# Up-projections of two channel mixers as seven block products for eight, woven between the down-projections

## Chip, cores, metric

One core of one Trainium2 chip. The metric is the device time of one execution in microseconds (us). Before the change it is 791.82 us, median of 3 executions (791.28 to 792.13).

## What is computed

`x` is the output of a clustered attention, 2 batches of 768 tokens with 512 features. Two mixer layers follow, each a token mixing and a channel mixing. All of it is float32.

```python
def _moe_ref(x, U, V, w_ch1, w_ch2):            # layer 1: w_ch1 512 x 2048, w_ch2 2048 x 512
    xt = x.transpose(0, 2, 1)
    h = xt @ U @ V
    u = x + h.transpose(0, 2, 1)
    ch = np.maximum(u @ w_ch1, 0.0) @ w_ch2
    return (u + ch).astype(np.float32)

def _moe2_ref(x, w_tok1, w_tok2, w_ch1, w_ch2): # layer 2: w_ch1 512 x 1536, w_ch2 1536 x 512
    xt = x.transpose(0, 2, 1)
    h = np.maximum(xt @ w_tok1, 0.0) @ w_tok2   # 768 -> 256 -> 768
    u = x + h.transpose(0, 2, 1)
    h2 = np.maximum(u @ w_ch1, 0.0) @ w_ch2
    return (u + h2).astype(np.float32)
```

## The kernel before

Everything runs in a format of TensorE with a reduced mantissa (`F32R`), so each operand is split into a high part (ScalarE, a copy that rounds) and a low part (VectorE, the value minus its high part), and each product is three matmuls: high by high, high by low, low by high. Engines are programmed one by one, each with its own instruction list, and meet only in semaphores (`wait_ge`, `then_inc`), so the order within an engine is the order in which its list is written.

`attention` fills the first 266 us or so. `mixers` (L774) does the rest. `x` stays in SBUF as 12 tiles of 128 tokens by 512 features, the first six those of batch 0. PSUM has eight banks: `hid` (2), `spare` (2), `acc` (4).

**Tokens.** `token_first(L)` (L944, matmuls L957) contracts over tokens; `token_second(L, i)` (L961, L976) brings tile i back to tokens, and VectorE adds it to x (L1117). In layer 1, VectorE first makes the low parts of batch 1's tiles (L1099). GpSimd (POOL) splits V and the two token weights (L906 to L919), and between the layers it splits x (L926, L928).

**Channels.** `channel(L)` (L979) goes over three chunks of 512 tokens. Four tiles are transposed on TensorE (L940) and split out of PSUM by ScalarE (L1043) and VectorE (L1094). Then come the hidden features, one tile f of 128 at a time: `up(f)` (L984, L989) is 4 feature tiles x 3 = 12 matmuls with 512 moving columns into one of two `hid` banks; ScalarE takes relu and the high part out of PSUM (L1067), VectorE the low part (L1126); `down(f)` (L993, L998) is 4 token tiles x 3 = 12 matmuls of 512 columns that accumulate in `acc` over all f. The order is up(f+1), down(f), up(f+2), and so on. The weights of tile f are loaded by SyncE (L882, L884) and split by ScalarE (L1039, L1069) and VectorE (L1089, L1130). At the end of a chunk VectorE adds `acc` to x (L1150). There are 84 pairs of a chunk and a tile f (3 x 16 and 3 x 12), so 1008 up matmuls and 1008 down matmuls. The loops over f are hardware loops.

Of the kernel before, what the change touches and what calls it, by code (L numbers as in the profile page):

```python
# [4 lines left out]
F32 = mybir.dt.float32  # L5
F32R = mybir.dt.float32r
I32 = mybir.dt.int32
ALU = mybir.AluOpType
# [765 lines left out]
def mixers(nc, x, hi, q_lo, ident, V_raw, uv_in, w_ch1, w_ch2, w_tok1, w_tok2, v_ch1, v_ch2, out):  # L774


    R2 = w_tok1.shape[1]
    NR = R2 // P
    NTT = B * NT
    TPC = CHUNK // P  # L780
    layers = [(w_ch1, w_ch2), (v_ch1, v_ch2)]
    with ExitStack() as ctx:
        def sb(name, shape, dt=F32):
            return ctx.enter_context(nc.sbuf_tensor(name, shape, dt))
# [4 lines left out]


        bank = [ctx.enter_context(nc.psum_tensor(f"bank{i}", [P, BANK], F32)) for i in range(8)]
        hid, spare, acc = bank[0:2], bank[2:4], bank[4:8]


        x_hi, x_lo = token_tiles(hi[0]), token_tiles(hi[1])
        uT_hi = [sb(f"uT_hi{i}", [P, KD, CHUNK], F32R) for i in range(2)]
        uT_lo = [sb(f"uT_lo{i}", [P, KD, CHUNK], F32R) for i in range(2)]
        w1_raw = [sb(f"w1_raw{i}", [P, KD, P]) for i in range(2)]
        w2_raw = [sb(f"w2_raw{i}", [P, DM]) for i in range(2)]
        w1_hi = [sb(f"w1_hi{i}", [P, KD, P], F32R) for i in range(2)]  # L800
        w1_lo = [sb(f"w1_lo{i}", [P, KD, P], F32R) for i in range(2)]
        w2_hi = [sb(f"w2_hi{i}", [P, DM], F32R) for i in range(2)]
        w2_lo = [sb(f"w2_lo{i}", [P, DM], F32R) for i in range(2)]
        h_hi = [sb(f"h_hi{i}", [P, CHUNK], F32R) for i in range(2)]
        h_lo = [sb(f"h_lo{i}", [P, CHUNK], F32R) for i in range(2)]


        U_st = q_lo[:, 0, :].rearrange("p (t c) -> p t c", t=NT)
        V_hi = q_lo[:, 1, :]
        V_lo = q_lo[:, 2, :]  # L810
        t1 = sb("t1", [4 * RANK, B, DM], F32R)

        wt1_raw = sb("wt1_raw", [P, NT, R2])
        wt1_hi, wt1_lo = (q_lo[:, at:at + 2, :].rearrange("p g s -> p (g s)").rearrange("p (t r) -> p t r", t=NT)
                          for at in (4, 6))
        wt2_raw = sb("wt2_raw", [P, NR, S])
        wt2_hi = sb("wt2_hi", [P, NR, S], F32R)
        wt2_lo = sb("wt2_lo", [P, NR, S], F32R)
        t2_hi = sb("t2_hi", [P, B * NR, DM], F32R)
        t2_lo = sb("t2_lo", [P, B * NR, DM], F32R)  # L820
# [3 lines left out]
        wt_made = sem("wt_made")  # L824
        w1_in = [sem(f"w1_in{i}") for i in range(2)]
        w2_in = [sem(f"w2_in{i}") for i in range(2)]
        w1_hi_made = sem("w1_hi_made")
        w1_made = sem("w1_made")
        w2_hi_made = sem("w2_hi_made")
        w2_made = sem("w2_made")  # L830
        h_hi_made = sem("h_hi_made")
        h_made = sem("h_made")
        uT_hi_made = sem("uT_hi_made")
        uT_made = sem("uT_made")
        x_hi_made = sem("x_hi_made")
        x_made = sem("x_made")
        hid_mm = sem("hid_mm")
        acc_mm = sem("acc_mm")
        y_made = sem("y_made")
# [5 lines left out]
        u_tr = sem("u_tr")  # L845
        out_stored = sem("out_stored")


        nf = [layers[L][0].shape[1] // P for L in range(2)]
        chunks = [(L, c) for L in range(2) for c in range(NCHUNK)]  # L850
        base = [sum(nf[l] for l, _ in chunks[:i]) for i in range(len(chunks))]
        TOKS = (B, B * NR)
# [4 lines left out]
        def bank_of(L, n):  # L857

            return spare[n] if L == 0 or n < NR else hid[n - NR]

        def transposed_tile(a, i):
            cc, k = i // TPC, i % TPC
            return a[cc % 2][:, :, k * P:(k + 1) * P]

        def on_chip_order(a, t0=0):
            return a.rearrange("r (p t) -> r t p", t=NT)
# [3 lines left out]

        block = ctx.enter_context(nc.Block())

        @block.sync
        def _(sp):
            for L, (wa, wb) in enumerate(layers):
                wa3 = wa.rearrange("(k p) f -> p k f", p=P)
                for c in range(NCHUNK):
                    n0 = base[L * NCHUNK + c]

                    def load(f, par):  # L880
                        wait(sp, w1_made, n0 + f - 1)
                        sp.dma_start(w1_raw[par][:, :, :], wa3[:, :, bass.ds(f * P, P)]).then_inc(w1_in[par], 16)  # L882
                        wait(sp, w2_made, n0 + f - 1)
                        sp.dma_start(w2_raw[par][:, :], wb[bass.ds(f * P, P), :]).then_inc(w2_in[par], 16)  # L884

                    load(0, 0)
                    load(1, 1)
                    if L == 0 and c == 0:
                        sp.dma_start(wt1_raw[:, :, :], w_tok1.rearrange("(p t) r -> p t r", t=NT)).then_inc(wt_in[0], 16)
                        sp.dma_start(wt2_raw[:, :, :], w_tok2.rearrange("(n p) s -> p n s", p=P)).then_inc(wt_in[1], 16)  # L890
                    with sp.Fori(0, nf[L] // 2 - 1) as i:
                        load(i * 2 + 2, 0)
                        load(i * 2 + 3, 1)
                    if L == 1 and c == NCHUNK - 1:

                        out_v = out.rearrange("b (p t) d -> b p t d", t=NT)
                        for i in range(NTT):
                            sp.wait_ge(y_made, NTT + i + 1)
                            sp.dma_start(out_v[i // NT, :, i % NT, :], tile_of(x, i)).then_inc(out_stored, 16)
# [301 lines left out]
```

## Time and profile before

| | |
|---|---|
| median of 3 executions | 791.82 us (791.28 to 792.13) |
| the profiled execution | 792.6 us |
| span of its profile | 790.7 us |
| TensorE (PE) busy | 768.8 us |
| VectorE (DVE), ScalarE (ACT), GpSimd (POOL) busy | 450.1, 361.7, 136.0 us |

The profile is of one execution. [...] PEld is the load of weights into the array. "Idle before" is the time for which an engine stood still ahead of a group. PEclk is the granted TensorE clock, 1.00 for 2.4 GHz and 0.50 for 1.2 GHz. Tensors that share an address are printed under one name of theirs (`kT_hi` in L1099 is `x_lo`, `qT_lo` in L908 is `V_lo`).

### The profile page before, as it was taken

The numbers are of one execution on the slowest core, as the hardware profiler recorded it, in microseconds if no ns is written. First come the engines' busy times: TensorE is split into PE (matmuls) and PEld (weight loads), VectorE is DVE, ScalarE is ACT, GpSimd is POOL, SyncE is SP. The second block draws the span as 40 slices with busy tenths as digits, with TensorE's granted clock in tenths as the row PEclk, the third lists the DMA queues.
The fourth block names the chain that finished last, engine by engine and source line by source line (L and its number), as shares of the span: only waits on it lengthen the run. The fifth ranks groups of instructions, "written<-read, shape, count | busy, mean of one in ns | idle before, by whom it ended". The sixth has DMA issues, their size and how long they took to land.

```text
span 790.7 us, 12902 instructions
## 1 busy us (share of the span) xinstructions
PE 768.8 (97%) x3997; PEld 659.8 (83%) x3997; DVE 450.1 (57%) x761; ACT 361.7 (46%) x742; POOL 136.0 (17%) x162
## 2 busy tenths in 40 slices
PE   7989999999999889999999999999999999999998
PEld 6878999999999668888888888888888888888886
DVE  4778999999999684333533353334254335334333
ACT  5567888888888533323333233332123233323321
POOL 1351332233228660000300040000300000000000
PEclk9999999999999999999999999999999999999999
DMA  7935354444441223333323323333003333333334
GB/s 246 225 105 134 94 122 103 119 105 119 105 117 33 70 96 101 93 105 83 104 80 106 99 84 110 88 98 106 0 1 107 93 93 94 93 106 84 103 105 173
DMA packets 82840, 81.08 MB, mean 103 GB/s; under 512 B 7296, under 2 KB 69056, under 8 KB 82816
## 3 DMA queue, kind: packets, MB, share of 16 engines
q1 hardware_dynamic: 82816, 80.77, 37.0%
q8 instruction: 14, 0.23, 0.1%
q14 instruction: 10, 0.08, 0.0%
HBM read 56.95 MB, written 4.72 MB: 78 GB/s over the span
## 4 chain that ended last, share of the span: by engine, by line
PE 63%; DVE 2%; ACT 0%; issue 0%
PE bank L998 29%; PE bank L989 29%; PE bank L976 2%; PE bank L957 2%; PE bank L940 1%; DVE kT_hi L1099 1%; DVE x L1117 0%; DVE x L1150 0%; DVE w_lo L1130 0%; DVE uT_lo L1094 0%; DVE w_lo L1089 0%; DVE t L1108 0%; DVE h_lo L1126 0%; ACT qT_hi L1048 0%; ACT h_hi L1067 0%
## 5 line engine op out<-in xcount | busy, mean ns | idle before, releaser
L1126 DVE SCALAR_TENSOR_TENSOR h_lo<-bank,h_hi 128x512 fp32r<-128x512 f32 x84 | 58.1, 692 | 261.8 <-ACT h_hi L1067 261.8
L1067 ACT ACTIVATE h_hi<-bank 128x512 fp32r<-128x512 f32 x84 | 50.2, 598 | 301.4 <-PE bank L989 301.4
L989 PE MATMUL bank<-uT_hi,w_hi 128*128 128x512 f32 x336 | 131.2, 391 | 0.0
L998 PE MATMUL bank<-w_hi,h_hi 128*128 128x512 f32 x336 | 131.1, 390 | 0.0
L989 PE MATMUL bank<-uT_hi,w_lo 128*128 128x512 f32 x336 | 130.8, 389 | 0.0
L989 PE MATMUL bank<-uT_lo,w_hi 128*128 128x512 f32 x336 | 130.8, 389 | 0.0
L998 PE MATMUL bank<-w_hi,h_lo 128*128 128x512 f32 x336 | 130.7, 389 | 0.0
L998 PE MATMUL bank<-w_lo,h_hi 128*128 128x512 f32 x336 | 130.7, 389 | 0.0
L595 DVE TENSOR_TENSOR pT_lo<-back,pT_hi 128x384 fp32r<-128x384 f32 x192 | 98.1, 552 | 6.9 <-ACT pT_hi L496 3.5
L496 ACT ACTIVATE pT_hi<-back 128x384 fp32r<-128x384 f32 x192 | 84.4, 497 | 36.2 <-PE back L740 34.6
L563 DVE TENSOR_REDUCE negmax<-front 128x1 f32<-128x768 f32 x96 | 91.3, 952 | 9.2 <-PE front L639 9.2
L447 ACT ACTIVATE prob<-front,negmax 128x768 f32<-128x768 f32 x96 | 87.9, 916 | 1.2 <-DVE negmax L563 1.2
L740 PE MATMUL back<-ident,prob 128*128 128x128 f32 x576 | 79.3, 274 | 0.4 <-DVE pT_lo L595 0.4
L989 PEld LDWEIGHTS bank<-uT_hi,w_hi 128*128 128x128 f32 x336 | 63.1, 188 | 13.5 <-DVE uT_lo L1094 0.4
L998 PEld LDWEIGHTS bank<-w_hi,h_hi 128*128 128x128 f32 x336 | 63.1, 188 | 13.2 <-issue 0.2
L998 PEld LDWEIGHTS bank<-w_hi,h_lo 128*128 128x128 f32 x336 | 63.1, 188 | 13.1
L989 PEld LDWEIGHTS bank<-uT_hi,w_lo 128*128 128x128 f32 x336 | 63.0, 188 | 13.1
L989 PEld LDWEIGHTS bank<-uT_lo,w_hi 128*128 128x128 f32 x336 | 63.1, 188 | 12.9
L998 PEld LDWEIGHTS bank<-w_lo,h_hi 128*128 128x128 f32 x336 | 63.1, 188 | 12.9
L740 PEld LDWEIGHTS back<-ident,prob 128*128 128x128 f32 x576 | 68.4, 141 | 2.7 <-DVE pT_lo L595 0.6
L758 PE MATMUL back<-pT_hi,v_split 128*128 128x384 f32 x192 | 67.9, 354 | 0.8 <-DVE pT_lo L595 0.6
L760 PE MATMUL back<-pT_lo,v_split 128*128 128x384 f32 x192 | 64.8, 337 | 0.0
(125 smaller groups left out, 1054.1 us busy)
## 6 DMA issues: line engine op xcount, KB each, us to landing
w_raw<-in_moe_w_ch_dram SPq DMA_DIRECT2D x168, 256.0 KB, 2.9
Q<-qT_hi SPq DMA_DIRECT2D x64, 96.0 KB, 2.2
K<-kT_hi SPq DMA_DIRECT2D x64, 96.0 KB, 2.1
q_raw<-in_q_dram SPq DMA_DIRECT2D x8, 384.0 KB, 6.0
k_raw<-in_k_dram SPq DMA_DIRECT2D x8, 384.0 KB, 7.0
Q<-qT_lo SPq DMA_DIRECT2D x32, 96.0 KB, 2.1
K<-kT_lo SPq DMA_DIRECT2D x32, 96.0 KB, 2.1
v_raw<-in_v_dram SPq DMA_DIRECT2D x16, 192.0 KB, 2.7
```

What stands on the lines that cost most here:

```text
L447: nc.scalar.activation(prob[t % 2][:, :], s_slot[t % 2], ACT.Exp, bias=negmax[:, t % TPP:t % TPP + 1], accum_out=sums[:, t % TPP:t % TPP + ...
L496: nc.scalar.activation(pT_hi[G % 2][:, HT * half:HT * half + HT, P * (t % GT):P * (t % GT) + P], t_bank[n % 3][:, 0:HT * P].rearrange("p ( ...
L563: nc.vector.tensor_reduce(negmax[:, t % TPP:t % TPP + 1], s_slot[t % 2], AX.X, ALU.max, negate=True).then_inc(max_done, 1)
L595: nc.vector.tensor_tensor(pT_lo[G % 2][own], t_bank[n % 3][:, 0:HT * P].rearrange("p (n c) -> p n c", c=P), pT_hi[G % 2][own].bitcast(F32) ...
L740: last = nc.tensor.transpose(t_bank[i % 3][:, t * P:(t + 1) * P], prob[n % 2][:, c:c + P], ident[:, :])
L758: nc.tensor.matmul(av_bank, v_sp[j][:, token_of(t), :], pT_hi[n % 2][:, t, :], start=(t == 0), stop=False)
L760: last = nc.tensor.matmul(av_bank, v_sp[j][:, token_of(t), :], pT_lo[n % 2][:, t, :], start=False, stop=(t == NT - 1))
L957: last = nc.tensor.matmul(bank_of(L, n)[:, :], w, y[:, i, :], start=(t == 0 and m == 0), stop=(t == NT - 1 and m == len(pairs) - 1))
L989: last = nc.tensor.matmul(hid[par][:, :], w[par][:, kd, :], y[cc % 2][:, kd, :], start=(kd == 0 and m == 0), stop=(kd == KD - 1 and m == 2))
L998: last = nc.tensor.matmul(acc[k][:, :], y[par][:, k * P:(k + 1) * P], w[par][:, :], start=(start and m == 0), stop=(stop and m == 2))
L1067: nc.scalar.activation(h_hi[par][:, :], hid[par][:, :], ACT.Relu).then_inc(h_hi_made, 1)
L1126: nc.vector.scalar_tensor_tensor(out=h_lo[par][:, :], in0=hid[par][:, :], scalar=0.0, in1=h_hi[par][:, :].bitcast(F32), op0=ALU.max, op1=A ...
```

## The change

The channel mixers work on four chunks of 768 tokens, one for each layer and batch (`cc` 0 to 3), and on pairs of hidden tiles (8, 8, 6 and 6 pairs, 28 in all; n is the pair's number in all of them, p that in its chunk). For one pair, the up-projection is a 2 x 2 by 2 x 2 block product: weights in halves of the features and two hidden tiles, activations in halves of the features and halves of the tokens (384 columns). It is formed with seven block products in place of eight (Winograd's form of Strassen's scheme), each of 2 x 3 = 6 matmuls of 384 columns.

- The weight sums (four, 128 x 256) are made by GpSimd (`pair_sums`), the activation sums (four, 128 x 768) by VectorE at the start of each chunk (`moving_sum`), between adding the last chunk's result to x (`settle`) and making low parts (`moving_low`, seven of 128 x 768 for a chunk).
- The products' results are put together by VectorE with seven adds of 384 columns (`combine`), each of a PSUM bank and something in SBUF; one product is first copied by ScalarE (`snapshot`). The hidden values now lie in SBUF (`h`), and are split from there with 768 columns at a time.
- Only two banks (`hid`) are left for products, so product q waits until q - 2 has been read; six banks are `acc`. After product q (1 to 6) of pair p come two of the twelve down units (3 matmuls each) of pair p - 1. A chunk's first pair has no pair before it; the last pair's down units run among the next chunk's transposes.
- Layer 2's token mixing of a batch is woven into the first two pairs of chunks 1 and 2 (`MIXED`), with x split by ScalarE and GpSimd (`stage_high`, `stage_low`).
- Every list is written out in full, without hardware loops. Many tensors of the mixers lie over attention's or each other's.

The diff, cut to its core (the removed side is the code above); first the constants, the wait for a bank, and GpSimd's list:

```diff
+    PRODS, COMBS, RING = 7, 7, 3
+    A_SLOT = (0, 1, 5, 2, 4, 6, 3)
+    READ_BY = (0, 1, 2, 3, 5, 6, 7)
+    BC_SUM = {2: 2, 3: 3, 4: 1, 6: 4}
+    UNITS = [(e, k) for e in range(2) for k in range(NT)]
+    MIXED = (1, 2)
+        acc, hid = bank[0:NT], bank[NT:]
...
+        def product_read(eng, n, q):
+            if q == 0:
+                eng.wait_ge(snap_done, n + 1)
+            else:
+                eng.wait_ge(comb_done, COMBS * n + READ_BY[q])
...
+            def pair_sums(n):
+                raw = a_raw[n % 2]
+                pool.wait_ge(w1_in[n % 2], (n // 2 + 1) * 32)
+                nc.gpsimd.tensor_tensor(raw[:, 4, :, :], raw[:, 2, :, :], raw[:, 3, :, :], ALU.add).then_inc(sums_made, 1)
...
+            def stage_low(m):
+                pool.wait_ge(st_hi_made, m + 1)
+                nc.gpsimd.tensor_tensor(x_lo[:, m % RING, :], tile_of(x, m), x_hi[:, m % RING, :].bitcast(F32),
+                                        ALU.subtract).then_inc(st_made, 1)
...
+            pair_sums(0)
...
+            pool.wait_ge(tok_mm, B)
+            for r in range(NR):
+                nc.gpsimd.tensor_copy(tiled(wt2_hi[:, r, :]), on_chip_order(wt2_raw[:, r, :])).then_inc(wt2_made, 1)
...
+            pair_sums(1)
+            for n in range(pbase[NCH]):
+                for cc in MIXED:
+                    if n == pbase[cc]:
+                        for t in range(NT):
+                            stage_low((cc - 1) * NT + t)
+                if n + 2 < pbase[NCH]:
+                    pair_sums(n + 2)
```

TensorE's list, after `token_second_low` and the first transposes:

```diff
+            for cc in range(NCH):
+                for p in range(npair[cc]):
+                    for q in range(PRODS):
+                        product(cc, p, q)
+                        if p > 0 and q > 0:
+                            down(cc, p - 1, 2 * q - 2)
+                            down(cc, p - 1, 2 * q - 1)
+                        if (cc, p, q) == (0, 0, 1):
+                            for t in range(NT // 2, NT):
+                                token_second_low(1, t)
+                        if cc in MIXED and p == 0 and q > 1:
+                            token_first(cc, q - 2)
+                            if q == PRODS - 1:
+                                token_first(cc, NT - 1)
+                        if cc in MIXED and p == 1 and q == 0:
+                            for t in range(NT):
+                                token_second(cc, t)
+                more = cc + 1 < NCH
+                for unit in range(len(UNITS)):
+                    if more and unit == 0:
+                        transpose_u(cc + 1, 0)
+                    if more and unit < NT - 1:
+                        transpose_u(cc + 1, unit + 1)
+                    down(cc, npair[cc] - 1, unit)
```

VectorE's list, after the low parts of batch 1's tiles, of `t1`, and six `add_mix`:

```diff
+            for part in range(2):
+                a_low(0, part)
+            for cc in range(NCH):
+                for p in range(npair[cc]):
+                    if p == 0:
+                        moving_low(cc, 0)
+                        moving_low(cc, 1)
+                        dve.wait_ge(uT_made, NT * (cc + 1))
+                        down_read(dve, n - 2, 1)
+                        moving_sum(cc, tmp2, block_of(0, 1), block_of(0, 0))
+                        dve.wait_ge(bc_sum, 4 * cc + 1)
+                        moving_sum(cc, tmp1, block_of(1, 1), tmp2)
+                        moving_sum(cc, block_of(0, 1), block_of(1, 1), block_of(0, 1))
+                        settle(cc, 0)
+                        moving_low(cc, 2)
+                        settle(cc, 1)
+                        moving_low(cc, 3)
+                    elif p == 1 and mixed:
+                        for t in range(NT):
+                            add_mix(cc + 1, t)
+                    combine(n, 1, c11, snap)
+                    combine(n, 2, c12, snap)
+                    if p == 0:
+                        dve.wait_ge(bc_made, PRODS * cc + 3)
+                        moving_sum(cc, tmp1, block_of(1, 0), tmp1)
+                        settle(cc, 2)
+                        moving_low(cc, 4)
+                    else:
+                        for e in range(2):
+                            w2_low(n, e)
+                        if more:
+                            a_low(n + 1, 0)
+                    combine(n, 3, c21, c12, 2)
+                    if p == 0:
+                        settle(cc, 3)
+                        moving_low(cc, 5)
+                    elif more:
+                        a_low(n + 1, 1)
+                    combine(n, 4, c22, c21, 3)
+                    combine(n, 4, c12, c12, 2)
+                    if p == 0:
+                        settle(cc, 4)
+                        moving_low(cc, 6)
+                        settle(cc, 5)
+                        for part in range(2):
+                            a_low(n + 1, part)
+                    combine(n, 5, c12, c12, 5)
+                    if p == 0:
+                        for e in range(2):
+                            w2_low(n, e)
+                    h_low(n, 0)
+                    combine(n, 6, c21, c21, 3)
+                    h_low(n, 1)
+                    if p == 0 and mixed:
+                        for r in range(NR):
+                            t2_low(cc, r)
```

Product q waits for `bc_made` (its moving low part) in a chunk's first pair, for `a_made` (both `a_low` of its pair) at q = 0, and for `product_read` of q - 2. ScalarE's list in a chunk's first pair is: six copies out of the transposes' banks with two `moving_high` after the third, then `moving_high` 2 to 6 with the snapshot after number 3, `stage_high` of six tiles among them in a mixed chunk (tile t after `settle` t), `a_high` of the next pair, the two `w2_high`, the two `h_high`, and in a mixed chunk `t2_high` twice. `token_second` waits for both `t2_low`.

## Rows read from the trace of the kernel before

**Rows 1.** Page, part 1: busy us and share by engine.

```profile
PE 768.8 (97%) x3997; PEld 659.8 (83%) x3997; DVE 450.1 (57%) x761; ACT 361.7 (46%) x742; POOL 136.0 (17%) x162
```

**Rows 2.** Chain that ended last, in order of time: start us, us, what.

```profile
298.64 2.72 PE bank L989 x12
...
380.24 0.87 PE bank L940 x8
...
553.48 16.32 PE bank L957 x72
```

**Rows 3.** Timeline of PE and PEld, attention's last group of 384 columns: start, us.

```profile
263.62 0.34 PE L760 MATMUL back<-pT_lo,v_split 128*128 128x384 f32 x1
263.62 0.19 PEld L758 LDWEIGHTS back<-pT_hi,v_split 128*128 128x128 f32 x1
...
265.38 0.33 PE L760 MATMUL back<-pT_lo,v_split 128*128 128x384 f32 x1
```

**Rows 4.** The same chain as in rows 2, from the mixers' start.

```profile
269.76 6.57 DVE kT_hi L1099 x6
...
279.09 3.68 DVE x L1117 x6
...
291.61 2.29 DVE w_lo L1130
...
295.87 2.77 PE bank L998 x12
```

**Rows 5.** Timelines of DVE, POOL, ACT, mixers' start and 470 to 473 us: start, us.

```profile
269.09 1.65 POOL L906 CAST qT_lo<-V_raw 128x768 fp32r<-128x768 f32 x1 [0.34 <-POOLq L95]
269.76 1.53 DVE L1099 TENSOR_TENSOR kT_hi<-x,qT_hi 128x512 fp32r<-128x512 f32 x1 [3.37 <-ACT qT_hi L1048]
270.82 2.55 POOL L908 TENSOR_TENSOR qT_lo<-V_raw,qT_lo 128x768 fp32r<-128x768 f32 x1
271.21 2.71 DVE L1099 TENSOR_TENSOR kT_hi<-x,qT_hi 128x512 fp32r<-128x512 f32 x1
275.31 0.63 ACT L1039 ACTIVATE w_hi<-w_raw 128x512 fp32r<-128x512 f32 x1 [0.87 <-DMA w_raw<-in_moe_w_ch_dram]
...
470.37 1.14 DVE L1130 TENSOR_TENSOR w_lo<-w_raw,w_hi 128x512 fp32r<-128x512 f32 x1
470.91 1.07 POOL L926 CAST qT_hi<-x 128x512 fp32r<-128x512 f32 x1
471.44 1.09 DVE L1089 TENSOR_TENSOR w_lo<-w_raw,w_hi 128x512 fp32r<-128x512 f32 x1
472.06 1.62 POOL L928 TENSOR_TENSOR kT_hi<-x,qT_hi 128x512 fp32r<-128x512 f32 x1
472.48 0.69 DVE L1126 SCALAR_TENSOR_TENSOR h_lo<-bank,h_hi 128x512 fp32r<-128x512 f32 x1
```

**Rows 6.** Groups by line and shape: xcount | busy us, mean ns | idle before.

```profile
L595 DVE TENSOR_TENSOR pT_lo<-back,pT_hi 128x384 fp32r<-128x384 f32 x192 | 98.1, 552 | 6.9 <-ACT pT_hi L496 3.5
L1089 DVE TENSOR_TENSOR w_lo<-w_raw,w_hi 128x512 fp32r<-128x512 f32 x84 | 57.5, 690 | 7.2 <-ACT w_hi L1039 7.2
L569 DVE SCALAR_TENSOR_TENSOR qT_lo<-back,qT_hi 128x768 fp32r<-128x768 f32 x8 | 7.6, 954 | 5.2 <-ACT qT_hi L465 5.2
L447 ACT ACTIVATE prob<-front,negmax 128x768 f32<-128x768 f32 x96 | 87.9, 916 | 1.2 <-DVE negmax L563 1.2
L385 POOL TENSOR_TENSOR avsum<-av 128x192 f32<-128x192 f32 x32 | 19.1, 598 | 130.9 <-ACT av L503 130.9
L913 POOL TENSOR_TENSOR qT_lo<-wt_raw,qT_lo 128x1536 fp32r<-128x1536 f32 x1 | 3.5, 3481 | 0.1
L919 POOL TENSOR_TENSOR wt_lo<-wt_raw,wt_hi 128x768 fp32r<-128x768 f32 x2 | 4.5, 2257 | 0.2
```

**Rows 7.** Windows: us, busy (x) of PE, PEld, DVE, ACT, POOL, PEclk, DMA.

```profile
266.00:269.00 3.00, 0.55 (x3) 0.31 (x3) 0.39 (x2) 0.49 (x1) 1.09 (x2) 1.00 0.00 0
270.30:273.60 3.30, 3.30 (x9) 2.58 (x9) 3.30 (x2) 2.03 (x4) 2.99 (x2) 0.52 0.59 183
```

More of the change, by code:

```diff
@@ new lines, in mixers @@
+        uT = sb("uT", [P, KD, S])
+        sb("wt1_area", [P, KD, S])
+        with ExitStack() as under:
+            sb("bc_area", [P, 2 * PRODS - 2, 2, GW], where=under)
+            wt2_raw = sb("wt2_raw", [P, NR, S], where=under)
+        bc_hi = sb("bc_hi", [P, PRODS, 2, GW], F32R)
+        bc_lo = sb("bc_lo", [P, PRODS, 2, GW], F32R)
+        with ExitStack() as under:
+            tmps = []
+            for n in range(2):
+                tmps.append(sb(f"moving_sum{n}", [P, 2, GW], where=under))
+                sb(f"moving_area{n}", [P, 2 * DM - 2 * GW], where=under)
@@ new lines, in flat_a, with rows @@
+        def flat_a(a):
+            return a[:, :, :, :].rearrange("p s k c -> p (s k c)")
+        def rows(a, first, count):
+            return a[:, first:first + count, :].rearrange("p n c -> p (n c)")
+        tmp2, tmp1 = (t[:, :, :] for t in tmps)
+        snap = V_raw[:, 0:GW]
+        V_hi, V_lo = (flat_a(a_hi[1])[:, i * S:(i + 1) * S] for i in range(2))
+        t1 = flat_a(a_lo[1])[:, 0:B * DM].rearrange("p (b c) -> p b c", b=B)
+        t2_hi, t2_lo = (a[:, RING:RING + NR, :] for a in (x_hi, x_lo))
@@ L874, in _ @@
         def _(sp):
[L875 to L899, printed above, removed]
@@ new lines, in token_second @@
+            def token_second(cc, t):
+                cols = slice(t * P, (t + 1) * P)
+                m = (cc + 1) * NT + t
+                ring = NT - NR
+                if t == 0:
+                    pe.wait_ge(wt2_made, 2 * NR)
+                    pe.wait_ge(tok_made, B + NR * cc)
+                    pe.wait_ge(y_made, cc * NT)
+                wait(pe, u_made, m - ring + 1 if t >= ring else 0)
+                for r in range(NR):
+                    for i, (w, y) in enumerate(((wt2_hi, t2_hi), (wt2_hi, t2_lo), (wt2_lo, t2_hi))):
+                        last = nc.tensor.matmul(acc[NR + t % ring][:, :], w[:, r, cols], y[:, r, :],
+                                                start=(r == 0 and i == 0), stop=(r == NR - 1 and i == 2))
+                last.then_inc(mix_mm, 1)
@@ L1153, in program @@
+            for k in range(NT):
+                add_down(NCH - 1, k)
 def program(nc, q, k, v, centroids, U, V, w_ch1, w_ch2, w_tok1, w_tok2, v_ch1, v_ch2, out):
```

581 lines of the change are left out of this document (335 added, 246 removed).

## Prediction

> **What bounds the kernel now.** I read the page's busy times first: TensorE is busy for 97% of the span, and the next engine for 57% [rows 1]. Then the chain of waits, in order of time: from 295.87 us to the end it is TensorE alone, 12 matmuls in 2.72 us again and again (226.7 ns for each 512 columns), eight transposes in 0.87 us (0.11 each), the written-out 72 matmuls of L957 at the same full pace (16.32 us) [rows 2]. So only fewer or shorter matmuls help, as long as nobody makes TensorE wait. The one part that TensorE does not set is the mixers' start: 26.8 us from 269.1 to the first down matmul at 295.87 [rows 4], holding 48 token matmuls (10.9 us), 24 up matmuls (5.4) and 32 transposes (3.5), 19.8 us of work. VectorE holds most of that chain [rows 4]. The change puts four such seams where there is one.
>
> **The saving.** Columns of 384 appear in attention: ten starts from 263.62 to 265.38 us, 176 ns each, though each has a weight load of 190 ns of its own [rows 3]. Up-projection before: 1008 x 226.7 ns = 228.5 us. After: 28 pairs x 7 products x 6 = 1176 matmuls x 176 ns = 207.0 us. **Saved: 21.5 us.** Down, token and transpose matmuls keep their numbers (1008, 192, 96). [...]
>
> **Prices.** VectorE takes 3.68 us for six adds of 512 in a row, 0.61 each [rows 4]; one alone lasts 0.55, 0.69 and 0.95 us at 384, 512 and 768 columns [rows 6]. In a row I take 0.64 for 512 with its wait, 0.9 for 768, 2.0 for the two `a_low` (1792 columns together), 0.55 for a `combine`. ScalarE takes 0.92 for 768 [rows 6]. GpSimd goes from 0.60 us at 192 columns to 3.48 at 1536 [rows 6], so by that line 0.75 for one weight sum of 256, 3.1 for a pair's four with their waits, 1.3 for a `stage_low`.
>
> **The lock.** A two-input VectorE instruction from SBUF waits while GpSimd works. L1099's first lasts 1.53 us beside the V_hi cast and its second 2.71, ending half a microsecond after V_lo; at 470 us they take turns: 1.14 and 1.09 us for VectorE instructions whose group has a mean of 0.69, with GpSimd's 1.07 and 1.62 between and after them. L1126, which reads PSUM, takes 0.69 beside a running GpSimd subtraction [rows 5, 6]. Before, most of VectorE's work in a seam reads PSUM. After, `moving_low`, `moving_sum`, `a_low`, `w2_low` and `h_low` all read SBUF twice. [...] The rows show turns.
>
> **Opening, chunk 0.** Six VectorE subtractions end at 276.33 [rows 4]; the four sums of `pair_sums(0)` now fall among the last of them, once the weights land at about 275 (the third load of before released ScalarE at 275.31 [rows 5]), and take two turns: 277.8. Then `t1` (no longer behind two `w1_low`) and six `add_mix`: 283.5. From there VectorE's list up to the first down matmul, if it never waited: two `a_low` 2.0; `moving_low` 0 to 6, 6.3; four `moving_sum` 3.6; six `settle` 3.9; six `combine` of pair 0 (q = 1 to 5, two of them for q = 4), 3.3; two `a_low` 2.0; two `w2_low` 1.3; `h_low` 0.9; `combine` 6, 0.55: 23.9 us, to 307.4, and product 1 of pair 1 (1.05) ends at 308.5. Meanwhile GpSimd has the rest of `wt1_lo` (3), the two casts and two subtractions of `wt2` (1.65 and 2.26 each, 7.8 in all [rows 5, 6]), and the sums of pairs 1 and 2 (6.2): 17 us, each instruction between two of VectorE's. Some 3.5 us of it lie beside `settle` and `combine`, which read PSUM. That leaves 13.5: **first down matmul at 322**. TensorE's work by then is 10.9 + 24 transposes 2.6 + 9 products 9.5 = 23.0 us. Beyond its work it takes 322 - 269.1 - 23.0 = 29.9 us, before 7.0. **Cost 22.9 us**; bounds 9.5 (GpSimd never in the way) and 27 (all of its time counts).
>
> **Chunks 1 and 2.** Count from the last pair's transposes, which alternate with its down units: TensorE is through with both at 11.2 us (24 x 0.11 + 36 x 0.2267 = 10.8, and 0.4 for two waits for copies). `uT` is complete at about 6.7, because two `moving_high` (0.9 each) stand between ScalarE's copies. From 6.7 VectorE needs: four sums 3.6, five `moving_low` 4.5, six `settle` 3.9, six `combine` 3.3, two `a_low` 2.0: 17.3, with 0.5 of waits for products 24.5. Six `stage_low` (1.3 each, 7.8) lie there too; half find PSUM work beside them: 28.4. TensorE fills the time with 7 products (7.4) and 36 `token_first` matmuls (8.2), to 26.8, so it waits some 1.6 us. After one more product, at 29.5, it stands before `token_second`, which waits for `t2_low`: VectorE still has two `w2_low`, `h_low`, `combine` 6 (2.8), `pair_sums` of the next pair take turns with them (3.1), then `h_high` 0.9, two `t2_high` 1.2 and the last `t2_low` 0.7: 36.4 to 37.1. What is late next is that one wait, and behind it nothing on TensorE can go. **Cost 8.3 us each**, 16.6; bounds 3.3 (no lock) and 11 each.
>
> **Chunk 3.** No token matmuls, no GpSimd work in the list: 24.5, then `w2_low`, `h_low`, `combine` 6 to 27.3, product 1 to 28.4. TensorE's nine products (9.5) fit in the 17.2 us after 11.2. **Cost 7.7**; bounds 6 and 10.
>
> **Inside a chunk.** A pair takes 42 x 0.176 + 36 x 0.2267 = 15.6 us. VectorE needs 7 x 0.55 + 1.3 + 2.0 + 1.8 = 9.0, with all of GpSimd's 3.1 before it 12.1; between a product and the one that wants its bank lie two units and a product (2.4 us), where `combine` needs 0.55 behind at most three other instructions. I cost it at nothing; its cover is those 3.5 us. SyncE issues `load_pair` of n + 2 after `a_low` of n and `load_w2` of n, in pair n - 1, so a pair ahead of GpSimd's use; at 15.6 us a pair nothing there either. Written-out code: the 72 matmuls of L957 are written out and run at full pace [rows 2]. The tail (last adds paced by units of 0.68 us) stays.
>
> **Clock.** TensorE was busy for 0.55 of 3 us, and then ran 3.3 us at a granted 0.52 (1.2 GHz) although busy throughout [rows 7]. Nine matmuls ran where full pace has 14.6, a loss of some 1.6 us. The seams' waits can do the same: once each in chunks 1 and 2, one and a half times in the opening, where a slow product is mostly hidden by VectorE. **Cost 4 us**, bounds 0 and 7.
>
> **Sum.** -21.5 + 22.9 + 16.6 + 7.7 + 4 = +29.7 on the profiled execution's 792.6, that is 822.3. It was 0.8 us above the median, so 821.5, some 3.7% slower.
>
> **Rivals.**
> - *GpSimd does not hold VectorE up* (it is served second, or its work falls into gaps). Then -21.5 + 9.5 + 6.6 + 6 + 0 to 2 = +1 to +3 us, 793 to 795, up to 800 with half of the lock. For it: L1126 and the other PSUM reads go untouched, and a GpSimd instruction between two waits of VectorE costs nothing; against it: the turns in rows 5. Chance 0.17, a third of it within 0.2%.
> - *Faster: the seams cost less than the saving.* It is decided at one point, the sum of the four seams' waits against 21.5 us. If VectorE ran its SBUF list at a third less than my prices, opening +5, chunks 1 and 2 +1 each, chunk 3 +4 give -10.5: 781. Against: 0.95 us for 768 columns in a row of 8 [rows 6]. For: the two mixed chunks have 8.2 us of token matmuls to fill in. Chance 0.14.
> - *Inside a chunk, too, a product waits for its bank*, because `combine` stands behind `w2_low` and `a_low` and these behind GpSimd. Half of the slack missed in 24 woven pairs, 1 us each: 846. Chance 0.08.
> - *The 384-column matmul gains nothing here*, its weight load of 190 ns being the pace: 1176 x 190 = 223, saving 5: 838. Rows 3 speak against it. Chance 0.03.
>
> My forecast keeps 0.58. Its own range is 805 to 836. Down to 787 it takes in the first rival, up to 838 a part of the others; about 2 in 10 is left out, most of it the faster rival. Faster or slower by 0.2% (1.6 us, about what a measurement of this kernel can tell) counts as a change: faster 0.15, same 0.06, slower 0.79.
>
> **What would show it.** In the changed kernel: products' matmuls start 176 ns apart; inside a chunk TensorE runs without gaps, 15.6 us a pair; the first down matmul stands near 322 us; in VectorE's groups the two-input SBUF instructions of the seams last longer than 0.95 us on average, those that read PSUM do not; `token_second` has the longest single waits, for `t2_low`; the clock dips after them. The forecast is wrong if the first down matmul stands before 310, if the waits before `token_second` are under 3 us, or if gaps appear inside chunks.

## The result, and the profile after

The changed kernel takes **819.39 us** (median of 4 executions, 816.92 to 822.90) against 791.98 (791.28 to 793.95) beside it: a ratio of **1.0345, 95% interval 1.0302 to 1.0389**. The profiled execution took 820.13 us, span 818.2, mean granted clock 0.970. The forecast was 821.5 and "slower".

The first parts of the page, to be laid beside [rows 1]:

```profile
PE 767.1 (94%) x4165; PEld 684.9 (84%) x4165; DVE 579.1 (71%) x893; ACT 386.0 (47%) x698; POOL 234.2 (29%) x262
```

TensorE's work hardly changed in busy time (768.8 before), since its recorded spans overlap (343 to 347 ns on average for a matmul of 384 columns, 173.6 from start to start) and some matmuls now run at half clock (granted 0.50); VectorE has 129 us more, GpSimd 98. What matters is where TensorE stands still. Its waits in the whole kernel, with total, number and longest (L1087 are the products, L1053 is `token_second`):

```profile
PE bank L1087 <- DVE bc_lo L1279: 12.8, 7, 3.8
PE bank L1053 <- issue: 10.8, 2, 5.4
PE bank L1087 <- DVE h L1299: 5.4, 4, 1.8
```

Products wait for `moving_low` (L1279) or for `combine` (L1299), the token matmuls twice for 5.4 us; "issue" means that the view names no releaser there.

**Inside a chunk** the chain of waits is TensorE alone: six matmuls of a product, six of two down units, in turn, and twelve where two products meet.

```profile
333.84 2.08 PE bank L1087 x12
335.92 1.39 PE bank L1101 x6
337.31 1.04 PE bank L1087 x6
...
349.48 2.08 PE bank L1087 x12
```

From 333.84 to 349.48 is one pair: 15.64 us. Before, two hidden tiles of 512 tokens took 4 x 2.72 us, and for 768 tokens that is 4 x 2.72 x 1.5 = 16.32 [rows 2]. The twelve matmuls of 384 columns take 2.083 us, 173.6 ns each.

**The opening.** Mixers start at 268.20 (the first split of a batch 1 tile, at 269.1 before [rows 4]); the first down matmul is at 318.42, 50.2 us later, against 26.8 before and 52.9 forecast. The chain of waits there, beginning and end:

```profile
268.89 8.17 DVE kT_hi L1303 x6
...
279.23 3.68 DVE x L1253 x6
282.91 4.58 DVE a_lo L1245 x2
287.49 5.11 DVE bc_lo L1279 x2
292.60 2.90 DVE moving_sum L1273
...
299.82 2.30 PE bank L1087 x6
...
305.66 2.30 PE bank L1087 x6
...
316.13 2.29 PE bank L1087 x6
318.42 2.56 PE bank L1101 x6
```

The first row is the subtractions that took 6.57 us in [rows 4]. `a_low` (L1245) takes 4.58 for two, two `moving_low` 5.11, one `moving_sum` (L1273) 2.90; the prediction had 2.0, 1.8 and 0.9. Three products take 2.30 us each, at half clock (granted 0.50 at all three), in place of 1.05. The order of time of both engines says why (start, length, instruction; the rows of the other engines are left out):

```profile
280.66 3.49 POOL L991 TENSOR_TENSOR qT_lo<-h,qT_lo 128x1536 fp32r<-128x1536 f32 x1
282.83 4.66 DVE L1245 TENSOR_TENSOR a_lo<-a_raw,a_hi 128x1024 fp32r<-128x1024 f32 x2
...
284.10 2.56 POOL L995 CAST qT_hi<-wt_raw 128x768 fp32r<-128x768 f32 x1
...
286.75 2.78 POOL L997 TENSOR_TENSOR kT_hi<-wt_raw,qT_hi 128x768 fp32r<-128x768 f32 x1
287.41 5.19 DVE L1279 TENSOR_TENSOR bc_lo<-uT,bc_hi 128x768 fp32r<-128x768 f32 x2
...
289.47 2.31 POOL L995 CAST qT_hi<-wt_raw 128x768 fp32r<-128x768 f32 x1
...
291.86 2.81 POOL L997 TENSOR_TENSOR kT_hi<-wt_raw,qT_hi 128x768 fp32r<-128x768 f32 x1
292.52 2.97 DVE L1273 TENSOR_TENSOR moving_sum<-uT 128x768 f32<-128x768 f32 x1
```

From 282.83 us on the ends of the two engines' records alternate, one of GpSimd's and one of VectorE's: GpSimd's at 284.15, 286.66, 289.53, 291.78 and 294.67, VectorE's at 285.24, 287.49, 290.34, 292.60 and 295.49. That is what this document calls turns. The two `moving_low` last 5.19 us (2.93 and 2.34) beside a subtraction of 2.78 and a cast of 2.31; each ends 0.8 us after the GpSimd instruction that was running when it started, and in chunk 3, with GpSimd idle, the same two take 1.83 us. The groups by shape show which instructions stretch:

```profile
L1299 DVE TENSOR_TENSOR h<-bank,h 128x384 f32<-128x384 f32 x140 | 75.0, 552 | 51.3 <-PE bank L1087 51.2
L1279 DVE TENSOR_TENSOR bc_lo<-uT,bc_hi 128x768 fp32r<-128x768 f32 x16 | 19.3, 1226 | 5.4 <-ACT bc_hi L1162 5.4
L1279 DVE TENSOR_TENSOR bc_lo<-moving_sum,bc_hi 128x768 fp32r<-128x768 f32 x12 | 11.3, 945 | 0.0
L1273 DVE TENSOR_TENSOR moving_sum<-uT 128x768 f32<-128x768 f32 x4 | 5.8, 1461 | 2.4 <-ACT uT L1152 2.4
```

Two SBUF inputs: up to 1461 ns on average (of the four first `moving_sum`, the opening's takes 2966 ns, the median is 959), and 945 in the group that does not stretch; in chunk 3, where GpSimd has nothing from 705 to 724 us, each alone takes 0.94 to 0.96 us and two in a row 1.83. One input in PSUM: 552, as before [rows 6].

**The mixed seam** of chunk 1 (chunk 2's is the same), from product (n+1, 0) on, in the chain of waits:

```profile
454.87 1.05 PE bank L1087 x6
455.92 5.39 issue
461.31 10.51 PE bank L1053 x36
```

and TensorE by stretches across it (after the stretch: length, busy time and count of PE, PEld, DVE, ACT and POOL, then the granted clock, DMA share, GB/s):

```profile
457.00:460.40 3.40, 0.00 (x0) 0.00 (x0) 2.49 (x4) 2.23 (x5) 1.25 (x1) 0.77 0.89 235
460.40:463.80 3.40, 2.49 (x6) 2.04 (x7) 0.80 (x2) 2.59 (x3) 2.34 (x4) 0.50 0.04 12
463.80:467.20 3.40, 3.40 (x12) 2.65 (x12) 1.38 (x2) 0.00 (x0) 0.50 (x1) 0.72 0.00 0
```

TensorE stands still for 5.4 us and comes back at a granted 0.50. There its matmuls of 512 columns start 0.427 us apart (461.87 to 464.86), in the opening's slow products those of 384 start 0.320 apart (300.31 to 301.91), both 1.2 columns a ns; at 1.00 the step from 384 columns (173.6 ns) to 512 (226.7) is 53.1 ns, 2.4 columns a ns. Counted as one column a cycle, these are the 1.2 and 2.4 GHz of the sections ahead. The 36 matmuls behind the wait take 10.51 us, in the second seam 10.90, where 36 x 0.2267 = 8.16 at the upper level in an unbroken row.

**Where the 27.5 us went**, from one profiled execution (792.6) to the other (820.13):

| term | forecast | measured |
|---|---|---|
| narrower matmuls | -21.5 | -21.5, and +1.5 (below) |
| mixers start | 0 | -0.9 |
| opening | +22.9 | +20.2 |
| chunks 1 and 2 | +16.6 | +12.4 of waits |
| chunk 3 | +7.7 | +8.2 |
| clock, outside the opening | +4 | +1.8 behind the opening, 2.4 and 2.7 behind the mixed waits |
| not placed | | +0.7 |
| sum | +29.7 | +27.5 |

The opening's 20.2 is 50.2 less 23.0 of work, against 7.0 before. A mixed seam's 6.2 is 461.31 - 427.67 (its first transpose), less 27.4 of work, and chunk 3's 8.2 is 28.56 less 20.3; the forecast had counted 0.4 us of waits for copies as work in each, so on its own terms each of these three seams is 0.4 smaller. Half-clock time lies inside the opening too, in its 20.2. VectorE is busy beside the first two slow products and stands still for 0.45 us at the end of each; nothing runs beside the third (2.29 for 1.05). That makes 2.1 us at most.

### The profile page after: what moved, and what is told of

Its sections match the earlier page's. It is cut to its first block, busy times and chain, and to the rows that moved or that the text cites. A ratio compares the mean times of both kernels' runs of the same rounds, so it can differ in the third digit from the quotient of the medians.

```text
span 818.2 us, 12517 instructions
## 1 busy us (share of the span) xinstructions
PE 767.1 (94%) x4165; PEld 684.9 (84%) x4165; DVE 579.1 (71%) x893; ACT 386.0 (47%) x698; POOL 234.2 (29%) x262
## 4 chain that ended last, share of the span: by engine, by line
PE 56%; DVE 8%; issue 3%; POOL 0%; ACT 0%; ACTq 0%
PE bank L1101 28%; PE bank L1087 23%; PE bank L1053 3%; DVE bc_lo L1279 2%; DVE h L1299 1%; PE bank L1069 1%; DVE a_lo L1245 1%; DVE kT_hi L1303 1%; DVE x L1258 1%; DVE x L1253 1%; DVE moving_sum L1273 1%; PE bank L1038 0%; POOL kT_hi L979 0%; DVE w_lo L1284 0%; DVE kT_hi L1289 0%
## 5 line engine op out<-in xcount | busy, mean ns | idle before, releaser
L1087 PE MATMUL bank<-bc_hi,a_hi 128*128 128x384 f32 x392 | 136.1, 347 | 18.2 <-DVE bc_lo L1279 12.8
L1087 PE MATMUL bank<-bc_lo,a_hi 128*128 128x384 f32 x392 | 135.3, 345 | 0.0
L1087 PE MATMUL bank<-bc_hi,a_lo 128*128 128x384 f32 x392 | 134.4, 343 | 0.0
L1101 PE MATMUL bank<-w_hi,kT_hi 128*128 128x512 f32 x336 | 133.7, 398 | 0.0
L1101 PE MATMUL bank<-w_lo,qT_hi 128*128 128x512 f32 x336 | 133.0, 396 | 0.0
L1101 PE MATMUL bank<-w_hi,qT_hi 128*128 128x512 f32 x336 | 132.6, 395 | 0.0
L1299 DVE TENSOR_TENSOR h<-bank,h 128x384 f32<-128x384 f32 x140 | 75.0, 552 | 51.3 <-PE bank L1087 51.2
L1087 PEld LDWEIGHTS bank<-bc_hi,a_hi 128*128 128x128 f32 x392 | 76.0, 194 | 29.7 <-DVE bc_lo L1279 15.9
L563 DVE TENSOR_REDUCE negmax<-front 128x1 f32<-128x768 f32 x96 | 91.2, 951 | 9.0 <-PE front L639 9.0
L1087 PEld LDWEIGHTS bank<-bc_lo,a_hi 128*128 128x128 f32 x392 | 76.2, 194 | 7.2
L1087 PEld LDWEIGHTS bank<-bc_hi,a_lo 128*128 128x128 f32 x392 | 76.1, 194 | 0.0
L1101 PEld LDWEIGHTS bank<-w_hi,kT_hi 128*128 128x128 f32 x336 | 63.3, 188 | 13.5
L1299 DVE TENSOR_TENSOR h<-bank,V_raw 128x384 f32<-128x384 f32 x56 | 31.2, 557 | 55.8 <-PE bank L1087 55.8
```

Source lines behind the costliest of these rows:

```text
L563: nc.vector.tensor_reduce(negmax[:, t % TPP:t % TPP + 1], s_slot[t % 2], AX.X, ALU.max, negate=True).then_inc(max_done, 1)
L1087: last = nc.tensor.matmul(up_bank(n, q), w[n % 2][:, A_SLOT[q], kt, :], y[:, q, kt, :], start=(kt == 0 and i == 0), stop=(kt == 1 and i == 2))
L1101: last = nc.tensor.matmul(acc[k][:, :], y[:, e, k * P:(k + 1) * P], w[n % 2][:, e, :], start=(start and i == 0), stop=(stop and i == 2))
L1299: nc.vector.tensor_tensor(dst, up_bank(n, q), other, ALU.add).then_inc(comb_done, 1)
```

## The experiments

Two theories stood against each other for each seam. **A**: the time is VectorE's list, lengthened by turns with GpSimd's instructions, and the place of what TensorE waits for in that list. **B**: it is something else, the list's length alone, TensorE's own work, or the clock. The mixers' start moves between executions, from 268.2 to 273.1 us, although all before it is the same code. From the 17th of attention's 96 row maxima (VectorE, L563) to the last is 174.8 to 174.9 us in every trace, and the 17th starts between 81.9 and 86.9 us, so the difference arises before it. So lengths are also given from the mixers' start to the end of the span: 521.6 before, 550.0 after. Ratios are to the kernel before.

### Take GpSimd's split of the second token weight away

```diff
-            for r in range(NR):
-                nc.gpsimd.tensor_copy(tiled(wt2_hi[:, r, :]), ...)
-                ...
-                nc.gpsimd.tensor_tensor(tiled(wt2_lo[:, r, :]), ..., ALU.subtract)...
```

> Left out: GpSimd's two casts and two subtractions of the second token weight in the opening (10.5 us as recorded in the changed kernel, 7.8 us alone), so layer 2's second token product uses leftovers. Theory (GpSimd and VectorE take turns, each GpSimd instruction stands between two of VectorE's): the first down matmul, at 318.4 us in the changed kernel, comes 6 to 8 us earlier, 311.5, and the whole about as much, 812 to 813. Rival (the opening is VectorE's own list, GpSimd costs nothing): the first down matmul stays within 1 us, and the time with it.

812.73 us, ratio 1.0250 (1.0221 to 1.0279). The first down matmul is at 312.81, 42.9 after the mixers' start at 269.94: **7.3 less**, which A had at 6 to 8. From the start, 540.1. Four GpSimd instructions of 10.5 us in all, none of which anyone on TensorE waits for before `token_second`, cost 7 us of the opening. Most of the other 2.6 us of the 9.9 since the start is clock: here the matmuls right behind the opening run at the full one (the first six down matmuls take 1.39 us at a granted 1.00, not 2.56 at 0.50).

### The same time on GpSimd, without SBUF reads

```diff
+            for r in range(NR):
+                for i in range(6):
+                    wait(pool, wt2_made, 6 * r + i)
+                    nc.gpsimd.memset((wt2_hi if i < 3 else wt2_lo)[:, r, :].bitcast(F32), 0.0)...
```

> GpSimd's four instructions for the second token weight are twelve fills of 768 columns instead (some 8 us, as long as the four were alone), which write SBUF and read nothing; layer 2's second token product then uses zeros. Theory (what takes turns is reading SBUF, not GpSimd's being busy): VectorE's two moving_low of the opening take 1.8 us in place of 5.1, and the first down matmul comes 6 to 8 us earlier, as where the four were left out. Rival (GpSimd's being busy, or the semaphores that its list reaches late, hold VectorE): no change against the changed kernel.

813.93 us, ratio 1.0271 (1.0247 to 1.0295); first down 41.4 us after the start, not later than without any split (42.9). The order of time, GpSimd and VectorE:

```profile
283.39 2.33 POOL L997 MEMSET qT_hi<- 128x768 f32 x3
283.62 2.08 DVE L1244 TENSOR_TENSOR a_lo<-a_raw,a_hi 128x1024 fp32r<-128x1024 f32 x2
...
285.62 1.82 DVE L1278 TENSOR_TENSOR bc_lo<-uT,bc_hi 128x768 fp32r<-128x768 f32 x2
...
285.78 2.33 POOL L997 MEMSET kT_hi<- 128x768 f32 x3
```

GpSimd is about as busy (four times 2.33 us), and two `moving_low` take 1.82 us instead of 5.19. So it is not GpSimd's being busy that holds VectorE here but its instructions that read SBUF: a `moving_low`, with its two SBUF inputs, takes 0.91 us beside fills against 2.6 beside casts and subtractions.

### Late settle, alone

In chunks 0 and 3, which have no token mixing, the six `settle` follow the last `combine` of the first pair instead of standing between the `moving_low`, and each of the first down units waits for its own `settle` only.

```diff
-                        settle(cc, 0)   # ... settle(cc, 5), between the moving_low
+                        if mixed:
+                            settle(cc, 0)
...
+                    for k in range(2, NT if late else 2):
+                        settle(cc, k)
```

> Only the late settle of chunks 0 and 3, in the changed kernel. Theory (list length): the six adds of 0.6 us leave the path but the first: in chunk 3 the first down matmul comes 3.3 us earlier (25.3 us behind the first transpose in place of 28.6). In chunk 0 less, since settle also lay beside GpSimd's turns, 0 to 3 us. 813 to 816 in all. Rival (products, not VectorE, set the seam): no change.

815.61 us, ratio 1.0283 (1.0260 to 1.0306). The first down matmul comes 46.1 us after the start (-4.1, expected 0 to -3), and chunk 3's 26.35 after its first transpose (-2.2, expected -3.3). VectorE's list is the limit in chunk 3 too, where GpSimd has nothing, but only from its first `combine` on. That one waits for product 1, in the changed kernel for 1.19 us and here for 2.25:

```profile
715.42 0.56 DVE L1299 TENSOR_TENSOR h<-bank,V_raw 128x384 f32<-128x384 f32 x1 [1.19 <-PE bank L1087]
712.80 0.56 DVE L1302 TENSOR_TENSOR h<-bank,V_raw 128x384 f32<-128x384 f32 x1 [2.25 <-PE bank L1087]
```

(the first row is the changed kernel's, the second this run's). The two `settle` ahead of it filled a wait for TensorE and had cost nothing; of the four behind it, 0.6 us each, 2.2 us come back.

### GpSimd's sums later in the mixed seams

```diff
                 if n + 2 < pbase[NCH]:
+                    for cc in MIXED:
+                        if n == pbase[cc]:
+                            pool.wait_ge(tok_made, B + NR * cc)
                     pair_sums(n + 2)
```

> In chunks 1 and 2 GpSimd makes the weight sums of the pair after next only when t2_low is through. Theory (turns): the wait ahead of token_second, 5.4 us twice, shrinks by the 3.1 us of the four sums to about 2.3 each; 6 us in all, 813. If the shorter wait also keeps the clock up, another 2.7 us for each. Rival (the wait is VectorE's and ScalarE's own chain of w2_low, h_low, combine, h_high, t2_high, t2_low): no change.

816.09 us, ratio 1.0301 (1.0259 to 1.0342). The wait is 4.2 us instead of 5.4: **-1.2, not -3.1**. The turns with the sums were a smaller part of this wait than I had it; the next run shows that the order of the lists is the larger. The matmuls behind the wait took 10.03 and 9.85 us. From the start the run is 4.9 us shorter, of which the two waits are 2.4; much of the rest is clock, here and behind the opening, whose code is the same.

### `t2` first in both lists

ScalarE makes `t2_high` ahead of `h_high`, VectorE `t2_low` ahead of `h_low` and the last `combine`; the sums wait as above.

```diff
-                        if mixed:            # ScalarE: h_high, then t2_high
+                    if mixed and p == 0:     # t2_high, then h_high
+                        for r in range(NR):
+                            t2_high(cc, r)
```

> In chunks 1 and 2 the two t2_high stand before h_high and the two t2_low before h_low, and GpSimd's sums of the pair after next wait for them. Theory (token_second waits for a chain that is late only by its place in the lists): the wait of 5.4 us goes to about 1, and the half clock behind it (2.7 us) goes with it, some 7 us for each, 805 to 807. Rival (the work put off comes back as a wait of the product behind token_second, and the clock falls anyway): 4 us or less for each, 811 or more.

809.26 us, ratio 1.0201 (1.0175 to 1.0228), above the 805 to 807 that A had. From the start, 536.75: **-13.2**, near A's 7 for each seam.

```profile
456.31 1.00 issue
457.31 2.76 PE bank L1056 x11
```

The wait is 1.0 us, and the 36 matmuls behind it take 8.43 us in both seams. Against 5.4 and 10.51 or 10.90, the place in the lists cost, with the sums' 1.2, 4.4 us of waiting and 2.1 to 2.5 of clock in each.

### Fill the wait with matmuls that nobody uses

```diff
                         if cc in MIXED and p == 1 and q == 0:
+                            for i in range(20):
+                                nc.tensor.matmul(acc[NT - 1][:, :], wt1_hi[:, i % NT, 0:P], ...)
```

> Twenty matmuls of 512 columns without use (4.5 us) ahead of each token_second, inside its wait of 5.4 us, into a bank that the next matmul there starts anew. Theory (the half clock behind the wait costs time of its own): the 36 matmuls of token_second take 8.2 us in place of 10.9, 2.7 us less each, 814 in all. Rival (the clock costs nothing that is not waited for anyway): no change within 1 us; if the fill ends after t2_low, up to 1 us slower each.

817.33 us, ratio 1.0299 (1.0268 to 1.0330), where 814 was expected; from the start 545.7, -4.3.

```profile
454.94 4.57 PE bank L1133 x20
459.51 0.81 issue
460.32 8.44 PE bank L1053 x36
```

`token_second` starts no earlier against the seam's own beginning (22.49 us after the down matmuls' end, as without them), but its 36 matmuls take **8.44 us instead of 10.51, and 8.43 instead of 10.90** in the second, at a granted 1.00 in both. The only thing that differs is what TensorE did before: 4.57 us of matmuls in place of standing still. So the clock is a cost of its own, 2.1 and 2.5 us (A had 2.7), and the wait is not TensorE's to shorten. The 0.27 us by which 8.43 exceeds 8.16 is not the clock's; the table's 2.4 and 2.7 hold it.

What the clock takes behind such a wait varies. Over all the runs of this document:

| wait before `token_second` | its 36 matmuls, us |
|---|---|
| 0.8 to 1.0 | 8.42 to 8.44 |
| 2.3 | 10.04, 10.05 |
| 4.2 | 9.85 to 11.27 |
| 5.3 to 5.4 | 9.79 to 11.23 |

A wait of 2.3 us already costs 1.6 us of clock, and one of 5.4 between 1.4 and 2.8.

### The first `a_low` of the next pair at the end of the last

```diff
-                        for part in range(2):
-                            a_low(n + 1, part)
+                        if cc == 0:
+                            ...
+                    if p == npair[cc] - 1 and cc + 1 < NCH:
+                        for part in range(2):
+                            a_low(n + 2, part)
```

> The low parts of a chunk's second pair of weights are made before the seam's activation work, while VectorE waits for the transposes (chunks 1 to 3). Theory (the seam is VectorE's list): chunk 3's first down matmul, 28.6 us behind its first transpose, comes 2.0 us earlier; in chunks 1 and 2, where a_low took 3.7 us in turns with GpSimd, 2 to 3.7; 6 to 9 us in all, 811 to 813. Rival (the seam is set by the products' order or by ScalarE's copies, which now start later): no change, or 1 us slower for each seam.

806.78 us, ratio 1.0162 (1.0132 to 1.0192), below the 811 to 813 that were expected. The four executions lie far apart, from 802.98 us (granted clock 0.985) to 814.60 (0.973), and the profile is of the slowest; from its start, 541.1, -8.9, inside the 6 to 9. Two us of VectorE's list less give 1.8 in chunk 3, and 3.1 of the wait in each mixed seam (2.28 for 5.39), more than they last alone; in the changed kernel they take 3.72 in the first mixed seam, in turns with GpSimd's work. ScalarE's high parts move along with them and now delay the seam's second transposes, so against the first transpose `token_second` comes 2.8 us earlier.

### All sums on VectorE: a miss

`pair_sums` moves from GpSimd to VectorE, 0.34 us a sum.

> All weight sums on VectorE (four of 256 columns, about 1.4 us a pair with waits) in place of GpSimd (3.1 us alone). Theory (turns): the opening loses 6.2 us of GpSimd turns and gains 1.4, first down matmul at 313 to 314; the waits ahead of token_second lose 3.1 us each; inside a chunk nothing changes, VectorE has 10.4 of 15.6 us. In all about 11 us less, 808. Rival (only VectorE's own list counts): 1.4 us more in the opening and in no place less, 820 to 822.

818.87 us, ratio 1.0317 (1.0282 to 1.0352); from the start 544.9, -5.1. The waits before `token_second` fell as they had with the sums put off, to 4.2. The opening gave 0.8 in place of 4 to 5, and the chain of waits shows a wait of my own making:

```profile
313.49 0.34 DVE a_raw L1242
313.83 0.02 issue
313.86 1.71 ACT a_hi L1133
```

The four sums for pair 1 stand late in VectorE's list, ScalarE's `a_high` (1.71 us) comes only behind them, and VectorE's `a_low` behind that. The run does not say what the sums' place is worth without that.

### Token weights off GpSimd: a miss, and why

ScalarE makes the high parts of both token weights, VectorE the low parts.

> In the opening GpSimd keeps only V and the sums of pairs 0 and 1, both after the low parts of x; ScalarE makes the high parts of the token weights, VectorE itself the low parts (3.4 us more in its list, 13 us of GpSimd turns less). Theory (turns): the first down matmul comes 39 to 41 us after the mixers' start in place of 50.2, and the whole is 10 to 12 us less, 808. Rival (the opening is as long as VectorE's list): 3 us later.

817.39 us, ratio 1.0312 (1.0286 to 1.0339); from the start 545.8, **-4.2 in place of -10 to -12**; the first down matmul comes 45.7 us after it, not 39 to 41. A new wait had taken the old one's place:

```profile
PE bank L1077 <- DVE bc_lo L1277: 8.7, 5, 3.7
PE bank L1077 <- ACT V_raw L1178: 4.8, 1, 4.8
```

I had put two strided copies (3.06 us together) ahead of `snapshot` (L1178) in ScalarE's list, and product 2 needs the bank that `snapshot` reads. How much of the shortfall this explains is not shown: no run moves these copies alone.

### Together, and then mended

Three of the moves go into one kernel: `t2` first, the early `a_low`, and the token weights off GpSimd.

> The three together. If their parts add up, 30 to 33 us less than the changed kernel: 786 to 789, under the 792 of before. Rival (each frees time that the same next wait takes back, the transposes and ScalarE's copies at the seams): half of it, 803 or more.

800.91 us, ratio 1.0103 (1.0082 to 1.0125); from the start 529.7, -20.3 (expected -30 to -33). The three alone gave 13.2, 8.9 and 4.2, 26.3 in all. The missing 6.0 fits a wait that was counted twice: the early `a_low` had taken 3.1 us off each, and `t2` first leaves only 1.0 of each, with or without it. With the copies behind `snapshot`, and the late settle:

> The three edits together, with ScalarE's snapshot put ahead of its two casts of the second token weight (product 2 waited 4.8 us for it), and in chunks 0 and 3 the six settle at the end of VectorE's seam list, each down unit waiting for its own. Theory (the seams are as long as VectorE's list): 1 us from the snapshot and 3.3 us in each of two seams, 793 in place of 800.9, the same as before the change. Rival (TensorE's own products are next in line there, with the clock at half): 2 us or less for each, 796 or more.

795.74 us, ratio 1.0038 (1.0027 to 1.0050); the first down matmul comes 41.8 us after the start (45.8 in the run before), and chunk 3's 24.9 after its first transpose (26.8). 793 was expected; the late settle gave 1.9 in chunk 3 where I had 3.3 again. Last, the fourth `moving_sum` goes ahead of the first `combine`, and GpSimd's sums for pair 2 wait until pair 0's adds are done:

> The last combination (795.7 us) with two more moves: the fourth moving_sum before the first combine, where VectorE stands still for 2.3 us in chunk 3, and GpSimd's sums for pair 2 only when pair 0 is put together, out of turns with the opening's list. Theory (the seams are VectorE's list and its turns): 3 us in the opening and 0.9 in each of four seams, 789 to 790, 0.3% under the kernel before the change. Rival (products at half clock and ScalarE's copies are what is left): 1 us or less in all, 795.

**792.31 us** (12 executions, 790.42 to 794.37) against 792.46 (17 executions, 790.92 to 794.12) of the kernel before: **ratio 1.0000, 0.9989 to 1.0011**. The 789 to 790 that were expected are missed: the opening became 1.3 us shorter and not 3, a mixed seam 0.4 and not 0.9, chunk 3 0.9. This version has the whole saving and has spent it exactly: beyond TensorE's work the opening still costs 10.5 us more than before, each mixed seam 1.9 and chunk 3 3.8, and the spacing of the matmuls 1.5, together 19.6 of the 21.5. The first down matmul is 40.5 us after the start; behind it TensorE waits this much to the end:

```profile
PE bank L1048 <- issue: 2.0, 2, 1.0
PE bank L1082 <- DVE bc_lo L1288: 1.1, 2, 0.6
PE bank L1082 <- DVE h L1308: 1.0, 1, 1.0
PE bank L1064 <- ACT uT L1150: 0.6, 3, 0.2
```

No version that ran beats the kernel before by more than its interval.

## Why the prediction was right, and where it was off

- **The saving: right.** Forecast 176 ns and 15.6 us a pair without gaps; measured 173.6 and 15.64. Beneath it lie two differences of opposite sign: 1176 x 2.4 ns = 2.8 us less for the narrow matmuls, and 864 x 5.0 ns = 4.3 more (24 woven pairs of 36), because a matmul of 512 columns takes 1.39 / 6 = 231.7 ns when it stands between narrow ones, 226.7 before [rows 2].
- **The lock: right in kind and place.** VectorE and GpSimd take turns in the opening where both read SBUF (5.19 us for two `moving_low`), VectorE's adds from PSUM keep their 0.55 us, and beside GpSimd's fills, which only write, the two `moving_low` took 1.82. Without the weight's split the opening is 7.3 us shorter. The first rival, in which GpSimd does not hold VectorE, is refuted by that run and by the turns at 282 to 292 us.
- **Opening: 2.7 us too much.** Forecast 52.9 from the start, measured 50.2. Larger errors lie beneath. From the last `add_mix` (282.91) to the last `combine` of pair 0 (316.09) VectorE needs 33.2 us. Its list by itself was priced at 23.9, and 0.9 are its waits for slow products, so the turns took 8.4 where I had 13.5: `wt1_lo` had 1.2 us left by then and not 3, and the rest of the difference is not split. Against that stand the 2.1 us of clock, which I had called mostly hidden.
- **Mixed seams: the wait is where it was forecast, 33.6 us after the first transpose in place of 36 to 37.** The step that was off is "`pair_sums` of the next pair take turns with them (3.1)": putting the sums off gave 1.2. The turns with `stage_low`, which I had at 3.9, were not tested by themselves. The rest is the list itself, and moving `t2` ahead in it took the wait from 5.4 to 1.0. My sum had a slip here too: 36.4 to 37.1 less 27.85 of work is 8.6 to 9.3 a seam, not 8.3.
- **Chunk 3: right.** 28.56 us to the first down matmul, forecast 28.4. In four runs whose lists are the same there (sums later, fill, `t2` first, token weights off GpSimd) it is 29.1 to 29.9, with the last product, partly or wholly at half clock, taking 1.9 to 2.3 us instead of 1.3; so some luck lies in the closeness.
- **Clock: the mis-sized term.** I priced it at 4 us (bounds 0 and 7) from one dip after a short pause, 1.6 us each. It came to 6.9 outside the opening, 2.4 and 2.7 behind the mixed waits and 1.8 behind the opening, and with up to 2.1 inside the opening it is past my upper bound. [rows 7] followed 2.4 us of standing still in 3, and I read a loss of 1.6 from the granted share; by its nine matmuls, where full pace has 14.6, it is 1.3. The price was too small in both places: 2.4 and 2.7 behind the mixed waits, up to 3.9 in and behind the opening. In the mixed seams it is a consequence of the wait: filled, or cut to 1.0 us, it is gone.
- **Sum.** The errors have both signs (opening -2.7, mixed waits -4.2, chunk 3 +0.5, clock +2.9, matmul spacing +1.5, start -0.9, not placed +0.7), and so the total is nearer than its parts, by luck: +27.5 measured, +29.7 forecast.
- **The rivals "faster", "bank waits inside a chunk" and "384 columns gain nothing"** fall by the same rows: 20.2 + 12.4 + 8.2 us of seams against 21.5, and no gap at all inside a chunk.

Still open: what in attention's first 87 us moves the mixers' start by up to 5 us between executions; why the same seam meets one dip of the clock in one run and two in another; and what a chunk's first pair would cost with eight plain block products, which need no activation sums. None of these was tried.

## What to carry to other kernels

A saving in each step of a loop is paid for at its seams: count how often the pipeline empties and refills, and price each refill by the list of the engine that has to prepare the first operands, before counting the saving. Where VectorE's list is the path, order it by what TensorE wants next (`t2` first, with GpSimd's sums later, took a wait of 5.4 us to 1.0), and keep casts and subtractions from SBUF off GpSimd there (four of them cost 7.3 us of the opening); here such moves, within the engines' lists and from one to another, took back all of the 27 us that the change had lost. The gains of two moves that shorten the same wait do not add. Price a wait of TensorE with the half-clock time behind it: 5.4 us of waiting cost 7.8 and 8.1 in the changed kernel, 7.0 to 8.5 over the runs.

## What the runs showed of the hardware beyond the forecast

- A matmul of 512 columns takes 231.7 ns between products of 384 columns and 226.7 among its own kind. The kernel before has the same where sixes of `token_second` stand between transposes (L976, from 577.04 us: six in 1.39); the cause was not isolated.
- After 5.4 us without work TensorE came back at a granted 0.50, and 36 matmuls of 512 columns took 10.90 us; after 4.57 us of unused matmuls and 0.81 us of waiting they took 8.44, and after 2.28 us of waiting 10.04.
- When VectorE and GpSimd both had SBUF reads to make, in the opening, they alternated instruction by instruction (4.66 for two, 2.56, 2.78, 5.19 for two, 2.31, 2.81), and neither got two in a row; GpSimd's sum of 256 columns lasts 1.3 to 1.5 us there (294.62 to 300.36 us), and 0.73 at 701.38 and 702.07 us.
- Reading 768 columns with a stride of six elements (`wt2_raw`, in the four runs that split it on these engines) took ScalarE 1.58 to 1.62 us and VectorE 1.51 to 1.54, against 0.85 and 0.95 in order.
